# Strided sparse attention and a rational MLP on one core: the whole program re-expressed as a dependency graph with a list schedule

## Chip, cores and metric

One core of a Trainium2 chip. The metric is device time in microseconds of one execution. The engines are TensorE (PE), VectorE (DVE), ScalarE (ACT), GpSimd (POOL) and SyncE (SP, which here only issues DMAs).

## The reference

Attention over `q`, `k`, `v` of shape (8 batches, 8 heads, 576 positions, 64), then an MLP on all 4608 tokens:

```
scores = (1/8) * q @ k.T
heads 0-3: keep 0 <= i-j < 32;  heads 4-7: keep j <= i and i % 32 == j % 32
x = softmax(scores) @ v          # heads concatenated: (4608, 512)
h = x @ w_in                     # (4608, 2048)
g = (a0 + a1 h + a2 h^2 + a3 h^3) / (1 + |b0||h| + |b1| h^2 + 1e-6)
out = g @ w_out                  # (4608, 512) float32
```

## The kernel before

Everything is bfloat16 on chip with float32 in PSUM. POOL casts q and k of a batch into DRAM scratch (L304, one DMA for a pair of heads) and v straight into SBUF (L289); SP then loads q and k transposed, a pair of heads per DMA (L316, L320). Three batches of v and four of q and k are cast ahead.

`attn_head` (one head) goes over five tiles of 128 keys. Scores stand with keys on partitions: a matmul of kT and qT (L371), a matmul that adds the mask through an identity (L384), Exp on ACT without a row maximum (L391), and matmuls with v (L407) that sum over key tiles in one PSUM bank; the 65th column of v is ones, so the row sum comes along. Local heads take some 192 or 256 queries per key tile, strided heads all queries from the key tile on, masked. DVE divides, one reciprocal and one multiplication for each block of tokens (L435, L443), into token tiles X of 128 rows. When a tile has all heads, SP transposes it in four DMAs of 128x128 (L481) into XT, 512 tokens to a chunk.

`mlp1` runs a chunk: 16 groups of four matmuls (L507), each copied out by ACT (L516). Then the Padé chain on 4 pieces of 2048 columns: seven DVE operations for denominator and numerator (L532 to L563), Ln and Exp(-x) on ACT as the division (L573, L581), two DVE operations for the product (L589, L594). `mlp2` runs four blocks of 16 matmuls with w_out into one PSUM bank (L626), copied by DVE (L636), stored by POOL (L645). There is one set of chain buffers (`NCS = 1`).

The order on each engine is the order in which the build loop emits: per batch eight heads, after each head one step of the waiting chain (Ln after head 5, Exp after head 6, the products after head 7), then the transposes, then `mlp2` of the last chunk and `mlp1` of the next. Each engine runs its list in order and waits on semaphores.

Of the kernel before, what the change touches and what calls it, by code (L numbers as in the profile page):

```python
# [6 lines left out]
AF = mybir.ActivationFunctionType  # L7

NEG_BIAS = -240.0
STRIDE = 32  # L10
P128 = 128

DEBUG_STAGE = None
ACT_SET_ID = 6
USE_ACT_PRELOAD = True
LIMIT_B = None
LIMIT_H = None
HEAD_LIST = None
CHAIN_G = None
LN_PER_TILE = False  # L20
XT_ON_ACT = False
# [9 lines left out]
class Ev:  # L31
    __slots__ = ("sig", "n")

    def __init__(self, sig, n):
        self.sig = sig
        self.n = n


class Sig:
    def __init__(self, nc, name, step=1):  # L40
        self.sem = nc.alloc_semaphore(name)
        self.step = step
        self.cnt = 0

    def reserve(self):
        self.cnt += 1
        return Ev(self, self.cnt)

    def cur(self):
        return Ev(self, self.cnt)  # L50


class EngQ:
    def __init__(self, name):
        self.name = name
        self.q = []
        self.maxwait = {}

    def waits(self, evs):
        need = []  # L60
        for ev in evs:
            if ev is None or ev.n <= 0:
                continue
            key = id(ev.sig)
            if self.maxwait.get(key, 0) >= ev.n:
                continue
            self.maxwait[key] = ev.n
            need.append(ev)
        return need


def _blocks(b, S):
    res = []
    u0 = b * S
    u_end = (b + 1) * S
    u = u0
    while u < u_end:
        g = u // P128
        u1 = min((g + 1) * P128, u_end)
        res.append((u - u0, u1 - u, g, u % P128))  # L80
        u = u1
    return res


def bass_strided_sparse_attn__then__act_rational_pade_kernel(nc, q, k, v, moe_w_in, moe_w_out, moe_a, moe_b, out):
    w_in, w_out, pa, pb = moe_w_in, moe_w_out, moe_a, moe_b
    B, H, S, D = q.shape
    assert D == 64
# [3 lines left out]
    assert w_in.shape[0] == Fin and w_out.shape[0] == Fmid  # L92
    NT = B * S
    assert out.shape[0] == NT and out.shape[1] == Fout
    assert S % 64 == 0 and NT % P128 == 0
    HL = H // 2

    NKT = (S + 127) // 128
    KT = [(t * 128, min(128, S - t * 128)) for t in range(NKT)]
    NPAIR = H // 2  # L100
    NK1 = Fin // 128
    NK2 = Fmid // 128
    NF = Fmid // 128
# [12 lines left out]
    A = nc.alloc_sbuf_tensor
    bfty = dt.bfloat16
    f32 = dt.float32
    VST = 68
    NLD = 3  # L120
    vb = [A(f"vb{i}", [128, NKT, H, VST], bfty) for i in range(NLD)]
    qs16 = nc.dram_tensor("qs16", [B, NPAIR, S, 128], bfty)
    ks16 = nc.dram_tensor("ks16", [B, NPAIR, S, 128], bfty)
    NQT = 6
    qT = [A(f"qT{i}", [128, NKT * 128], bfty) for i in range(NQT)]
    kT = [A(f"kT{i}", [128, NKT * 128], bfty) for i in range(NQT)]
    NE = 6
    ET = [A(f"ET{i}", [128, 512], bfty) for i in range(NE)]
    NXR = 8
    XR = [A(f"X{i}", [128, Fin], bfty) for i in range(NXR)]  # L130
    NXTS = 2
    XT = [[A(f"XT{c}_{kk}", [128, CH], bfty) for kk in range(NK1)] for c in range(NXTS)]
    NCS = 1
    HB = [A("hbt", [128, NF, CH], bfty)]
    QM = [A("qmt", [128, NF, CH], bfty)]
    LG = [A("lgt", [128, NF, CH], bfty)]
    T3B = [A("t3t", [128, NF, CH], bfty)]
    NLANE = 1
    ch_z = [A(f"chz{i}", [128, G, CH], bfty) for i in range(NLANE)]
# [650 lines left out]
```

How the kernel before makes its waits and increments, by code:

```python
def bass_strided_sparse_attn__then__act_rational_pade_kernel(nc, q, k, v, moe_w_in, moe_w_out, moe_a, moe_b, out):  # L85
# [116 lines left out]
        def thunk(eng, _need=need, _ev=ev, _maker=maker):  # L202
            for w in _need:
                eng.wait_ge(w.sig.sem, w.n * w.sig.step)
            inst = _maker(eng)
            inst.then_inc(_ev.sig.sem, _ev.sig.step)
# [255 lines left out]
    def do_x_transposes(g):  # L462
        xslot = g % NXR
        c = (g * P128) // CH
        cs = c % NXTS
        col0 = (g * P128) % CH
        if DEBUG_STAGE == 'x':
            ev = emit(QPOOL, S_dbg,
                      lambda s, xslot=xslot, g=g: s.dma_start(
                          out[g * 128:g * 128 + 128, 0:min(Fin, Fout)], XR[xslot][:, 0:min(Fin, Fout)]),
                      waits=[X_last_norm[g]])
            QPOOL.q.append(lambda p, ev=ev: p.wait_ge(ev.sig.sem, ev.n * ev.sig.step))
            X_free[xslot] = ev
            xt_done_ev[g] = ev
            return
# [268 lines left out]
    if DEBUG_STAGE is None:  # L744
        while pending_mlp2:
            run_steps(("dve", "ln", "exp"), 10 ** 6)
            mlp2(pending_mlp2.pop(0))
        run_steps(("dve", "ln", "exp"), 10 ** 6)
        while deferred_out:
            deferred_out.pop(0)[1]()
    for so in S_out:
        if so.cnt > 0:
            QPOOL.q.append(lambda p, so=so: p.wait_ge(so.sem, so.cnt * so.step))
    with nc.Block() as block:
        block.sync(lambda e: [f(e) for f in QSP.q])
```

## Time and profile before

| | |
|---|---|
| median of 3 runs (lowest to highest) | 925.08 us (922.75 to 926.25) |
| profiled execution, first to last instruction | 924.9 us |
| mean granted TensorE clock | 0.724 of 2.4 GHz |
| DMA | 180,868 packets, 42.73 MB |

Busy time is the time in which an engine runs instructions; SPq and POOLq are the queues' own work of issuing DMAs, which the page does not count as busy. A chain row is one link of the work that ended last, followed back from the end. Two matmuls in a row overlap, so a single matmul's mean is longer than its share of a row of them. No time of the profiled execution beyond its span is given.

### The profile page before, as it was taken

The page shows a single profiled execution, that of the slowest core. Times are in us where ns is not written, and L with a number is a line of the kernel's source. Part 1 is how long each engine was busy: PE and PEld are TensorE (multiplying, and loading weights), DVE is VectorE, ACT ScalarE, POOL GpSimd, SP SyncE. Part 2 cuts the span into 40 slices and gives each one's busy share as a digit, 9 for nine tenths or more (in the row PEclk, how much of TensorE's full clock was granted, in tenths as well). Part 3 has the DMA queues.
Part 4 walks back from the last instruction along what each step waited for, and adds up shares of the span by engine and source line. Part 5 has one row for each costly group of instructions (what it writes and reads, how often), then busy time and mean ns, then how long its engine had stood idle before and what let it go on. Part 6 is the DMA issues. An engine that isn't in the chain of part 4 may idle for free.

```text
span 924.9 us, 7533 instructions
## 1 busy us (share of the span) xinstructions
PE 593.8 (64%) x2704; PEld 255.2 (28%) x2704; DVE 460.7 (50%) x1001; ACT 345.3 (37%) x569; POOL 154.4 (17%) x167
## 2 busy tenths in 40 slices
PE   0493496469744985499628974698549854915706
PEld 0241142224321342134213432244213421302202
DVE  0131059522954098416941495319540984393681
ACT  0131155406460437124531555053704371261540
POOL 9986000240006000600020000000000000000000
PEclk9999975589556955596559755795569555967959
DMA  9999901490109010931051010101010000100001
GB/s 120 137 156 192 99 19 20 36 116 25 26 8 128 24 26 13 94 71 26 14 49 59 13 26 16 50 24 25 0 46 23 1 1 18 57 0 23 23 0 45
DMA packets 180868, 42.73 MB, mean 46 GB/s; under 512 B 175712, under 2 KB 178016, under 8 KB 180832
## 3 DMA queue, kind: packets, MB, share of 16 engines
q0 software_dynamic: 118016, 27.80, 30.7%
q1 hardware_dynamic: 62816, 14.47, 9.4%
q8 instruction: 21, 0.34, 0.2%
q14 instruction: 15, 0.12, 0.0%
HBM read 36.98 MB, written 18.87 MB: 60 GB/s over the span
## 4 chain that ended last, share of the span: by engine, by line
PE 53%; DVE 23%; ACT 15%; SPq 3%; DMA 2%; issue 2%; POOL 2%; DVEq 0%; POOLq 0%
PE ps_out L626 16%; PE ps_h L507 14%; PE ps_score L371 8%; PE ps_score L384 8%; PE ps_acc L407 7%; ACT lgt L573 7%; ACT qmt L581 5%; DVE lgt L594 5%; DVE chz L589 3%; DVE X L443 3%; ACT ET L391 3%; DVE outsb L636 2%; SPq L481 2%; DVE qmt L543 1%; DVE chu L554 1%
## 5 line engine op out<-in xcount | busy, mean ns | idle before, releaser
L626 PE MATMUL ps_out<-Wout,lgt 128*128 128x512 bf16 x576 | 148.2, 416 | 152.0 <-DVE lgt L594 130.8
L391 ACT ACTIVATE ET<-ps_score 128x192 bf16<-128x192 f32 (+5 forms) x352 | 126.6, 369 | 225.0 <-PE ps_score L384 195.5
L516 ACT ACTIVATE hbt<-ps_h 128x512 bf16<-128x512 f32 x144 | 86.0, 597 | 309.4 <-PE ps_h L507 309.4
L435 DVE RECIPROCAL rcol<-ps_acc 128x1 f32<-128x1 f32 (+1 forms) x320 | 51.1, 160 | 268.5 <-PE ps_acc L407 266.8
L407 PE MATMUL ps_acc<-vb,ET 128*128 128x65 bf16 (+3 forms) x784 | 127.0, 244 | 79.0 <-ACT ET L391 76.2
L371 PE MATMUL ps_score<-qT,kT 64*128 64x192 bf16 (+5 forms) x352 | 129.2, 367 | 28.7 <-DMA kT<-ks 28.7
L626 PEld LDWEIGHTS ps_out<-Wout,lgt 128*128 128x128 bf16 x576 | 57.8, 106 | 239.9 <-DVE lgt L594 132.7
L407 PEld LDWEIGHTS ps_acc<-vb,ET 128*128 128x128 bf16 (+3 forms) x784 | 75.7, 118 | 136.1 <-ACT ET L391 99.0
L636 DVE COPY outsb<-ps_out 128x512 f32<-128x512 f32 x36 | 24.9, 692 | 151.6 <-PE ps_out L626 151.6
L645 POOL DMA_DIRECT2D out_dram<-outsb x36 | 19.7, 548 | 468.3 <-DVE outsb L636 468.3
L443 DVE TENSOR_SCALAR X<-ps_acc,rcol 128x64 bf16<-128x64 f32 (+1 forms) x320 | 90.8, 284 | 11.4
L289 POOL DMA_DIRECT2D vb<-in_v_dram x40 | 36.3, 939 | 289.2 <-PE ps_acc L407 289.2
L304 POOL DMA_DIRECT2D ks<-in_k_dram x32 | 80.5, 4383 | 4.0 <-issue 4.0
L384 PE MATMUL ps_score<-MS,IDN 128*128 128x512 bf16 (+2 forms) x192 | 78.1, 407 | 0.9
L304 POOL DMA_DIRECT2D qs<-in_q_dram x32 | 77.0, 3952 | 3.4 <-issue 3.4
L573 ACT ACTIVATE lgt<-qmt,consts 128x2048 bf16<-128x2048 bf16 x36 | 69.4, 1990 | 15.9 <-DVE qmt L543 15.9
L507 PE MATMUL ps_h<-XT_0,Win 128*128 128x512 bf16 x144 | 55.3, 384 | 28.9 <-DMA XT_3<-X 28.9
L581 ACT ACTIVATE qmt<-lgt 128x2048 bf16<-128x2048 bf16 x36 | 65.6, 1896 | 0.0
L507 PE MATMUL ps_h<-XT_1,Win 128*128 128x512 bf16 x144 | 55.3, 384 | 0.0
L507 PE MATMUL ps_h<-XT_2,Win 128*128 128x512 bf16 x144 | 55.3, 384 | 0.0
L507 PE MATMUL ps_h<-XT_3,Win 128*128 128x512 bf16 x144 | 55.3, 384 | 0.0
L371 PEld LDWEIGHTS ps_score<-qT,kT 64*128 64x128 bf16 (+1 forms) x352 | 36.5, 104 | 65.6 <-DMA kT<-ks 28.8
(27 smaller groups left out, 496.6 us busy)
## 6 DMA issues: line engine op xcount, KB each, us to landing
out_dram<-outsb POOLq DMA_DIRECT2D x36, 256.0 KB, 2.3
qs<-in_q_dram POOLq DMA_DIRECT2D x32, 144.0 KB, 9.2
ks<-in_k_dram POOLq DMA_DIRECT2D x32, 144.0 KB, 9.5
vb<-in_v_dram POOLq DMA_DIRECT2D x32, 128.0 KB, 4.7
Win<-in_moe_w_in_dram POOLq DMA_DIRECT2D x4, 512.0 KB, 16.5
Wout<-in_moe_w_out_dram POOLq DMA_DIRECT2D x16, 128.0 KB, 22.0
XT_0<-X SPq DMA_TRANSPOSE x36, 3.1
XT_1<-X SPq DMA_TRANSPOSE x36, 2.4
```

Source lines behind the costliest of these rows:

```text
L304: lambda p, b=b, pair=pair, src_t=src_t, dst_t=dst_t: p.dma_start(dst_t[b, pair, :, :].rearrange("s (hh d) -> s hh d", hh=2), src_t[b, 2 * ...
L371: e.matmul(ps[0:nk, 0:x1 - x0], kT[tslot][pbase:pbase + 64, tk0:tk0 + nk], qT[tslot][pbase:pbase + 64, x0:x1], start=True, stop=False),
L384: e.matmul(ps[0:nk, 0:W], IDN[0:nk, 0:nk], mrhs, start=False, stop=True),
L391: a.activation(ET[esl][0:nk, 0:W], ps[0:nk, 0:W], AF.Exp, scale=0.125),
L407: return e.matmul(acc[rb:rb + M, VST * j:VST * j + 65], ET[esl][0:nk, ov0 - x0:ov0 - x0 + M], vb[slot][0:nk, ktile, h, 0:65], start=False, ...
L435: d.reciprocal(rcol[rl][r0:r0 + ns, 0:1], acc[r0:r0 + ns, VST * j + 64:VST * j + 65]),
L443: d.tensor_scalar(XR[xslot][r0:r0 + ns, h * D:(h + 1) * D], acc[r0:r0 + ns, VST * j:VST * j + 64], rcol[rl][r0:r0 + ns, 0:1], None, op0=Al ...
L507: e.matmul(psh[:, 0:CH], Win[kk][:, f * 128:(f + 1) * 128], XT[cs][kk][:, 0:CH], start=(kk == 0), stop=(kk == NK1 - 1)),
L516: a.activation(hbT[:, f, :], psh[:, 0:CH], AF.Copy),
L573: lambda a, qmT=qmT, lgT=lgT, f0=f0: a.activation(lgT[:, f0:f0 + G, :], qmT[:, f0:f0 + G, :], AF.Ln, bias=eps1_ap, scale=1.0),
L581: lambda a, qmT=qmT, lgT=lgT, f0=f0: a.activation(qmT[:, f0:f0 + G, :], lgT[:, f0:f0 + G, :], AF.Exp, scale=-1.0),
L626: e.matmul(pso[:, 0:Fout], LG[0][:, kk, m * 128:(m + 1) * 128], Wout[kk][:, 0:Fout], start=(kk == 0), stop=(kk == NK2 - 1)),
```

## The change

The order is no longer written by hand. Each step is put down as an `Op` with an engine, an assumed duration, a priority key (tokens) and the tiles it reads and writes; `schedule` plays the graph through with these durations, at each engine taking the ready step with the smallest key, and so fixes each engine's list at build time; `emit` writes the lists with the waits that are needed. The lists are static: each engine still runs its own in order.

Attention now has queries on partitions. A local head is six tiles of 96 queries by 128 keys, in two PSUM banks; strided heads go in pairs, each as six blocks by two parities of 54x54 (three residues of 18 tokens). Masks are put in first by matmul; DVE takes the row maximum, TensorE subtracts it through an identity, ACT does one Exp for the unit, SP transposes the probabilities from SBUF, TensorE multiplies with v, and DVE divides with one reciprocal and one multiplication. There are four local units and two strided ones per batch. Strided results go through DRAM (`xs16`, written by POOL) to be reordered; x is transposed by SP from SBUF (local, 256 columns at once) and from DRAM (strided). v is cast into DRAM and loaded by SP, 6 loads for local and 32 for strided heads per batch.

The MLP's chain runs in groups of 8 x 512 = 4096 columns, two per chunk, in rings of 6 (h), 2 (z) and 2 (u) buffers; its formulas are the same. Output blocks are copied by ACT instead of DVE. All casts of all batches depend on nothing and go out as early as their keys let them. Everything of the old body, `Sig`, `EngQ` and `_blocks` is removed. The core of what is added (a step's arguments after its function are assumed duration, key, reads `r`, writes `w`, changes `m`, and assumed transfer time `dma`):

```diff
+            t, e = best
+            while pend[e] and pend[e][0][0] <= t:
+                _, k, i, o = heapq.heappop(pend[e])
+                heapq.heappush(avail[e], (k, i, o))
+            _, _, o = heapq.heappop(avail[e])
+            free[e] = t + o.dur
+            if o.dma is not None:
+                dmafree = max(dmafree, t + o.dur) + o.dma
+                o.fin = dmafree + 2.2
+            else:
+                o.fin = t + o.dur
...
+                lat = 0.07 if u.eng == o.eng else 0.15
+                u.ready = max(u.ready, o.fin + lat)
...
+    R_pL = ring("pL", 3, [128, NTL * 128])
+    R_pS = ring("pS", 2, [128, 2 * NBK * 64])
+    R_ptL = ring("ptL", 2, [128, NTL, TQ])
+    R_ptS = ring("ptS", 2, [128, 2 * 3, 128])
...
+    R_xt = ring("xt", 3, [128, NK1, CH])
+    R_h = ring("h", 6, [128, G, CH])
+    R_z = ring("z", 2, [128, G, CH])
+    R_u = ring("u", 2, [128, G, CH])
...
+    R_ps = Ring([Tile(f"ps{i}", ps(f"ps_s{i}", [128, 2, 512])) for i in range(2)])
+    R_pa = Ring([Tile("pa0", ps("ps_acc", [128, 512]))])
+    R_ph = Ring([Tile(f"ph{i}", ps(f"ps_h{i}", [128, 512])) for i in range(2)])
+    R_po = Ring([Tile("po0", ps("ps_out", [128, 512]))])
...
+    def casts(b):
+        key = b * 576 - 1500 if b else -1e5
...
+        def local(pair):
+            for s_t, d_t in ((q, lq), (k, lk)):
+                P.op("pool", lambda e, s_t=s_t, d_t=d_t: e.dma_start(
+                    d_t[b, pair, :, :].rearrange("s (hh d) -> s hh d", hh=2),
+                    s_t[b, 2 * pair:2 * pair + 2, :, :].rearrange("hh s d -> s hh d")),
+                    4.0, key, w=[T_lqk[b]], dma=2.4)
...
+        def bulk(s_t, d_t, h0, t):
+            n = (H - h0) * S * D
+            c = 1024
+            P.op("pool", lambda e: e.dma_start(
+                bass.AP(tensor=d_t, offset=b * n, ap=[[c, n // c], [1, c]]),
+                bass.AP(tensor=s_t.tensor, offset=s_t.offset + (b * H + h0) * S * D, ap=[[c, n // c], [1, c]])),
+                1.2, key, w=[t], dma=0.9 * (H - h0) / 4)
...
+    def loads(b):
+        key = b * 576 - 700
...
+                P.op("sp", lambda e, t=t, d_t=d_t, pair=pair: e.dma_start_transpose(t.t[:, 0:S], d_t[b, pair, :, :]),
+                     0.15, key + pair, r=[T_lqk[b]], w=[t], dma=0.85)
...
+        for i in range(NTL):
+            w0 = max(0, TQ * i - STRIDE)
+            P.op("sp", lambda e, i=i, w0=w0: e.dma_start(
+                vl.t[:, i, :, 0:64], vs[b, 0:HL, w0:w0 + 128, :].rearrange("h p d -> p h d")),
+                0.15, key + 5, r=[T_v[b]], w=[vl], dma=0.7)
...
+                P.op("sp", lambda e, t=t, d_t=d_t, h=h: e.dma_start_transpose(
+                    t.t[:, h, 0:S // 2], d_t[b, h, :, :].rearrange("(c two) d -> c (two d)", two=2)),
+                    0.15, key + 10, r=[T_sqk[b]], w=[t], dma=0.43)
...
+                P.op("sp", lambda e, i=i, par=par, blk=blk, base=base: e.dma_start(
+                    vS.t[base:base + 52:3, blk // 2, par, :, blk % 2, 0:64],
+                    bass.AP(tensor=vs, offset=((b * H + HL) * S + 2 * i + par) * D,
+                            ap=[[32 * D, TT], [S * D, HL], [1, D]])),
+                    0.15, key + 12, r=[T_v[b]], w=[vS], dma=0.1)
...
+        for kind, idx in (("L", 0), ("S", 0), ("L", 1), ("S", 2), ("L", 2), ("L", 3)):
+            key = base + 96 * u
+            u += 1
+            sc = R_ps.next()
...
+                    for j, n in ((0, 4), (1, 2)):
+                        e.matmul(pst[0:TQ, j, 0:n * 128], IDN[:, 0:TQ], ML[:, j * 512:j * 512 + n * 128],
+                                 start=True, stop=False, skip_group_check=True)
...
+                    for i in range(NTL):
+                        w0 = max(0, TQ * i - STRIDE)
+                        c0 = (i % 4) * 128
+                        r = e.matmul(pst[0:TQ, i // 4, c0:c0 + 128],
+                                     tq.t[pb_:pb_ + 64, TQ * i:TQ * i + TQ], tk.t[pb_:pb_ + 64, w0:w0 + 128],
+                                     start=False, stop=True, skip_group_check=True)
+                    return r
...
+                flat = pst[0:TQ, :, :].rearrange("p a (t c) -> p (a t) c", c=128)[:, 0:NTL, :]
+                P.op("dve", lambda e, flat=flat, ng=ng: e.tensor_reduce(
+                    ng.t[0:TQ, 0:NTL], flat, axis=AX.X, op=Alu.max, negate=True), 0.97, key, r=[sc], w=[ng])
...
+                        r = e.matmul(pst[0:TQ, j, 0:n * 128], IDN[0:TQ, 0:TQ],
+                                     ng.t[0:TQ, 4 * j:4 * j + n].unsqueeze(2).broadcast_to([TQ, n, 128]),
+                                     start=False, stop=True, skip_group_check=True)
...
+                pp = R_pL.next()
+                P.op("act", lambda e, pp=pp, flat=flat: e.activation(
+                    pp.t[0:TQ, :].rearrange("p (t c) -> p t c", c=128), flat, AF.Exp, scale=0.125),
+                    0.83, key, r=[sc], w=[pp])
+                pt = R_ptL.next()
+                P.op("sp", lambda e, pp=pp, pt=pt: e.dma_start_transpose(pt.t[:, :, :], pp.t[0:TQ, :]),
+                     0.15, key, r=[pp], w=[pt], dma=0.83)
...
+                        r = e.matmul(acc.t[0:TQ, 65 * i:65 * i + 65], pt.t[:, i, :], vl.t[:, i, h, 0:65],
+                                     start=True, stop=True, skip_group_check=True)
...
+                P.op("dve", lambda e, rc=rc, a3=a3: e.reciprocal(rc.t[0:TQ, 0:NTL].unsqueeze(2), a3[:, :, 64:65]),
+                     0.22, key, r=[acc], w=[rc])
+                P.op("dve", lambda e, rc=rc, a3=a3, h=h: e.tensor_tensor(
+                    xl.t[0:TQ, :, 64 * h:64 * h + 64], a3[:, :, 0:64],
+                    rc.t[0:TQ, 0:NTL].unsqueeze(2).broadcast_to([TQ, NTL, 64]), op=Alu.mult),
+                    0.56, key, r=[acc, rc], w=[xl])
...
+                for j in range(2):
+                    e.matmul(pst[:, j, 0:NBK * 64], IDN[:, :], MS[:, :], start=True, stop=False,
+                             skip_group_check=True)
+                for j in range(2):
+                    for blk in range(NBK):
+                        for par in range(2):
+                            kc = tk.t[64 * par:64 * par + 64, idx + j, 3 * blk:3 * blk + 288]
+                            r = e.matmul(pst[64 * par:64 * par + SB, j, 64 * blk:64 * blk + SB],
+                                         tq.t[64 * par:64 * par + 64, idx + j, blk, :],
+                                         kc.rearrange("p (t i) -> p t i", i=16)[:, :, 0:3],
+                                         start=False, stop=True, skip_group_check=True)
...
+                    for g in range(3):
+                        for par, c0, mm in ((0, 0, 64), (1, 64, SB)):
+                            r = e.matmul(acc.t[c0:c0 + mm, 130 * g:130 * g + 130],
+                                         pt.t[0:NR, 3 * j + g, c0:c0 + mm], vS.t[0:NR, g, par, h, :, :],
+                                         start=True, stop=True, skip_group_check=True)
...
+                p0 = 64 * par + i3
+                P.op("pool", lambda e, p0=p0, nb=nb, i3=i3, par=par: e.dma_start(
+                    bass.AP(tensor=xs, offset=(b * S + 2 * i3 + par) * 256, ap=[[32 * 256, TT], [6 * 256, nb], [1, 256]]),
+                    xsb.t[p0:p0 + 52:3, 0:nb, :]), 1.0, base + 500, r=[xsb], w=[T_xs[b]], dma=0.4)
...
+                P.op("sp", lambda e, t=t, r0=r0, n=n, col=col, i=i: e.dma_start_transpose(
+                    t.t[:, 0:2, col:col + n], xl.t[r0:r0 + n, i, :]), 0.15, key + i, r=[xl], w=[t], dma=0.3)
...
+            P.op("sp", lambda e, t=t, r0=r0, n=n, col=col: e.dma_start_transpose(
+                t.t[:, 2:4, col:col + n], xs[b, r0:r0 + n, :]), 0.15, key + 10, r=[T_xs[b]], w=[t], dma=1.5 * n / 512)
...
+        base = c * CH + 1150
+        groups = []
+        for g in range(NG):
+            h = R_h.next()
+            for f in range(g * G, g * G + G):
+                ph = R_ph.next()
+                key = base + f * 16
...
+            P.op("act", lambda e, uu=uu: e.activation(uu, uu, AF.Ln, bias=eps1, scale=1.0),
+                 0.833 * W / 1000 + 0.28, key, r=[T_co], m=[u])
...
+        base = c * CH + 1900
+        for m in range(CH // 128):
+            po = R_po.next()
...
+            P.op("act", lambda e, o=o, po=po: e.activation(o.t[:, :], po.t[:, :], AF.Copy), 0.6, base + m * 60,
+                 r=[po], w=[o])
```

## Rows read from the trace of the kernel before

**Rows 1.** The page: span; then busy us, share and instruction count of each engine
```profile
span 924.9 us, 7533 instructions
...
PE 593.8 (64%) x2704; PEld 255.2 (28%) x2704; DVE 460.7 (50%) x1001; ACT 345.3 (37%) x569; POOL 154.4 (17%) x167
```

**Rows 2.** Windows: busy us (count), granted clock, DMA share in two stretches
```profile
core 0: us, PE busy (x) PEld busy (x) DVE busy (x) ACT busy (x) POOL busy (x), PEclk, DMA share, GB/s
128.00:193.00 65.00, 38.65 (x170) 16.98 (x170) 48.99 (x106) 27.48 (x44) 14.19 (x13) 0.50 0.45 43
193.00:227.00 34.00, 31.50 (x155) 12.92 (x152) 4.43 (x14) 12.13 (x24) 4.00 (x6) 1.00 0.40 57
```

**Rows 3.** Chain that ended last, in order of time: start us, us, what
```profile
208.23 13.83 PE ps_h L507 x64
...
251.14 7.57 ACT lgt L573 x4
...
294.16 3.64 PE ps_out L626 x16
```

**Rows 4.** Lines by shape, DVE chain: busy us, mean ns of one; idle before
```profile
L543 DVE TENSOR_TENSOR qmt<-chu,chz 128x2048 bf16<-128x2048 bf16 x36 | 44.1, 1226 | 1.2
...
L589 DVE TENSOR_SCALAR chz<-t3t,coef 128x2048 bf16<-128x2048 bf16 x36 | 29.8, 829 | 3.5 <-DVE lgt L594 0.5
...
L538 DVE TENSOR_SCALAR chu<-chz,coef 128x2048 bf16<-128x2048 bf16 x36 | 29.3, 813 | 1.3
...
L549 DVE TENSOR_SCALAR chz<-hbt,coef 128x2048 bf16<-128x2048 bf16 x36 | 29.2, 812 | 1.3
...
L558 DVE TENSOR_SCALAR chz<-chu,coef 128x2048 bf16<-128x2048 bf16 x36 | 27.1, 753 | 1.3
...
L532 DVE TENSOR_SCALAR chz<-hbt 128x2048 uint16<-128x2048 uint16 x36 | 24.6, 683 | 7.4 <-ACT hbt L516 6.8
```

**Rows 5.** Lines by shape, DVE in attention and output: busy us, mean ns
```profile
L435 DVE RECIPROCAL rcol<-ps_acc 128x1 f32<-128x1 f32 x256 | 40.8, 159 | 132.9 <-PE ps_acc L407 131.9
...
L636 DVE COPY outsb<-ps_out 128x512 f32<-128x512 f32 x36 | 24.9, 692 | 151.6 <-PE ps_out L626 151.6
```

**Rows 6.** Lines by shape, ACT: busy us, mean ns of one; idle before
```profile
L516 ACT ACTIVATE hbt<-ps_h 128x512 bf16<-128x512 f32 x144 | 86.0, 597 | 309.4 <-PE ps_h L507 309.4
...
L573 ACT ACTIVATE lgt<-qmt,consts 128x2048 bf16<-128x2048 bf16 x36 | 69.4, 1990 | 15.9 <-DVE qmt L543 15.9
...
L581 ACT ACTIVATE qmt<-lgt 128x2048 bf16<-128x2048 bf16 x36 | 65.6, 1896 | 0.0
...
L391 ACT ACTIVATE ET<-ps_score 128x512 bf16<-128x512 f32 x32 | 18.8, 588 | 40.3 <-PE ps_score L384 40.3
```

**Rows 7.** Timeline of SP's queue: start us, us, engine, line, operation
```profile
1.16 0.42 SPq L218 DMA_DIRECT2D MS<-c_ms  x1
1.62 0.42 SPq L219 DMA_DIRECT2D IDN<-c_idn  x1
...
28.59 1.20 SPq L316 DMA_TRANSPOSE qT<-qs  x1
29.84 1.27 SPq L320 DMA_TRANSPOSE kT<-ks  x1
...
85.97 1.23 SPq L481 DMA_TRANSPOSE XT_0<-X  x1
87.24 1.23 SPq L481 DMA_TRANSPOSE XT_1<-X  x1
```

**Rows 8.** Line L481: DMA time from issue to landing
```profile
DMA to landing us min/median/max: 2.2/2.6/11.1
```

**Rows 9.** Timeline of the start: first q/k cast, first score matmul
```profile
13.98 1.50 POOL L304 DMA_DIRECT2D qs<-in_q_dram  x1
...
35.87 0.39 PE L371 MATMUL ps_score<-qT,kT 64*128 64x256 bf16 x1 [28.69 <-DMA kT<-ks]
```

**Rows 10.** Chain that ended last, its last wait
```profile
915.34 3.86 issue
```

More of the change, by code:

```diff
@@ L85, in bass_strided_sparse_attn__then__act_rational_pade_kernel, with __init__, next @@
+class Ring:
+    def __init__(self, tiles):
+        self.tiles = tiles
+        self.i = 0
+    def next(self):
+        t = self.tiles[self.i % len(self.tiles)]
+        self.i += 1
+        return t.new()
 def bass_strided_sparse_attn__then__act_rational_pade_kernel(nc, q, k, v, moe_w_in, moe_w_out, moe_a, moe_b, out):
@@ L211, in _act_table_preload, with sb, ring @@
-    def _act_table_preload(a):
+    G = 8
+    NG = NF // G
+    TQ = 96
+    NTL = S // TQ
+    TT = S // STRIDE
+    NBK = 6
+    SB = 3 * TT
+    NR = 64 + SB
+    bf = dt.bfloat16
+    f32 = dt.float32
+    u16 = dt.uint16
+    P = Prog(nc)
+    def sb(name, shape, ty=bf):
+        return nc.alloc_sbuf_tensor(name, shape, ty)
+    def ring(name, n, shape, ty=bf):
+        return Ring([Tile(f"{name}{i}", sb(f"{name}{i}", shape, ty)) for i in range(n)])
+    lq = nc.dram_tensor("lq16", [B, 2, S, 128], bf)
@@ new lines, in bass_strided_sparse_attn__then__act_rational_pade_kernel @@
+    ki = np.arange(128)[None, :]
+    ml = np.full((128, NTL, 128), NEG, np.float32)
+    for i in range(NTL):
+        d = qi - ki if i == 0 else qi + STRIDE - ki
+        ml[:, i, :] = np.where((d >= 0) & (d < STRIDE), 0.0, NEG)
+    ms = np.full((128, NBK, 64), NEG, np.float32)
+    for half in (0, 64):
+        for a in range(SB):
+            for c in range(SB):
+                if a % 3 == c % 3 and c // 3 <= a // 3:
+                    ms[half + a, 0:5, c] = 0.0
+                    if a % 3 == 0:
+                        ms[half + a, 5, c] = 0.0
+            if a % 3:
+                ms[half + a, 5, a] = 0.0
@@ new lines, in mlp2, with mm @@
+    def mlp2(c, groups):
+        base = c * CH + 1900
+        for m in range(CH // 128):
+            po = R_po.next()
+            for g in range(NG):
+                def mm(e, m=m, g=g, po=po):
+                    r = None
+                    for j in range(G):
+                        kk = g * G + j
+                        r = e.matmul(po.t[:, :], groups[g].t[:, j, m * 128:(m + 1) * 128], Wout[:, kk, :],
+                                     start=(kk == 0), stop=(kk == NF - 1))
+                    return r
+                P.op("pe", mm, 0.216 * G, base + m * 60, r=[groups[g], T_wout], w=[po])
+            o = R_o.next()
+            P.op("act", lambda e, o=o, po=po: e.activation(o.t[:, :], po.t[:, :], AF.Copy), 0.6, base + m * 60,
+                 r=[po], w=[o])
+            u0 = c * CH + m * 128
+            dst = Tile(f"st{o.name}") if not hasattr(o, "st") else o.st
+            o.st = dst
+            dst.new()
+            P.op("pool", lambda e, o=o, u0=u0: e.dma_start(out[u0:u0 + 128, :], o.t[:, :]), 0.6, base + m * 60,
+                 r=[o], w=[dst], dma=0.9)
@@ L212, in _act_table_preload, with table @@
+    casts(0)
+    weights()
+    for b in range(1, B):
+        casts(b)
+    nxt = 0
+    st = loads(0)
+    pend = []
+    for b in range(B):
+        cur = st
+        if b + 1 < B:
+            st = loads(b + 1)
+        xl = attention(b, cur)
+        gather(b, xl)
+        while nxt < NCH and (nxt + 1) * CH <= (b + 1) * S:
+            gr = mlp1(nxt)
+            mlp2(nxt, gr)
+            nxt += 1
+    P.schedule()
+    def table(a):
         inst = mybir.InstLoadActFuncSet(name=nc.get_next_instruction_name(), ins=[], outs=[],
-                                         act_func_set_id=ACT_SET_ID)
+                                        act_func_set_id=ACT_SET_ID)
```

1105 lines of the change are left out of this document (430 added, 675 removed).

## The prediction

> **What bounds the kernel now.** I read the page's busy times first, then the windows of one period, then the chain that ended last. The page shows that no engine is full: TensorE is busy 64% of 924.9 us, DVE 50%, ACT 37% [rows 1]. So the span is made of turns. The chain shows whose: in one period the 64 matmuls of a chunk's first layer run alone for 13.83 us, later four Ln take ACT 7.57 us before anything of that chunk can go on, later four blocks of 16 output matmuls run alone at 3.64 us each [rows 3]; the next chunk starts only behind them, because each chunk has one buffer for its whole Padé chain. The windows show the two faces of the period: 65 us with attention and the Padé chain together, in which DVE is busy 49.0 us and TensorE is granted 0.50 of its clock (1.2 GHz), then 34 us of dense matmuls at 1.00 (2.4 GHz) with DVE busy 4.4 us [rows 2]. The gain to be had is to let DVE work in those 34 us; the question is what then becomes the limit. The profiled execution's span is 924.9 us, the median of the runs 925.08 us: the sum below is made against the span and 0.2 us more changes nothing. About 0.5% is what a measurement of this kernel can tell from no change.
>
> **The parts, by engine.** All counts come from the diff; a batch is 576 tokens, a chunk 512, so a batch has 1.125 chunks.
>
> *DVE, Padé chain.* Before, a piece of 2048 columns takes four tensor-tensor operations of 1226 ns and five tensor-scalars of 829, 813, 812, 753 and 683 ns, 8.79 us [rows 4]. The same nine now run on 4096 columns. Fixed cost of one: the 128x1 reciprocal's 159 ns [rows 5]. So one group costs 2 x 8.79 - 9 x 0.159 = 16.2 us (17.6 us if nothing is saved), 18 groups 291 us, with gaps 297 us. Before it was 36 x 8.79 = 317 us.
>
> *DVE, attention.* The row maximum does not exist in the trace. The nearest row is the copy of 128x512 out of PSUM, 692 ns, against 159 ns for one column: 1.04 ns a column [rows 5]. A maximum over 768 columns is then 0.96 us, over 648 columns 0.83 us, a normalisation of 384 columns 0.56 us and a reciprocal 0.17 us. A batch has four local heads (0.96 + 0.17 + 0.56) and two strided pairs (0.83 + 2 x 0.73): 11.3 us, with gaps 11.9 us, 95 us in all. Bounds for the maximum: free of the second bank's latency 0.7 us, twice the copy 1.4 us, which moves the total by +-20 us. The output copies go to ACT. DVE total: 297 + 95 + some 10 us of memsets at the start = 402 us, 49 us a batch.
>
> *ACT.* Ln 1990 ns and Exp 1896 ns at 2048 columns, against 588 ns at 512, give 0.85 ns a column [rows 6]; at 4096 they cost 3.7 and 3.6 us. Per chunk 2 x 7.3 + 16 x 0.597 + 4 x 0.6 = 26.6 us; attention has 4 x 0.80 + 2 x 0.70 = 4.6 us a batch. Sum 276 us, 35 us a batch. It stays off the bound.
>
> *TensorE.* The two layers keep their 1152 matmuls of 512 columns. At full clock they cost 13.83/64 = 0.216 and 3.64/16 = 0.228 us each [rows 3], 256 us together; at half clock 0.427 us, 492 us. Attention has per batch 4 x 2694 + 2 x 4392 = 19,560 columns, 8.2 us at 2.4 GHz and 16.3 us at 1.2 GHz, plus some 4 us for 144 short instructions. So a batch needs 43 us of TensorE at full clock, 81 us at half clock. The mean granted clock decides; the windows show it low whenever attention's short matmuls are in the stretch and high when the 512-column ones run alone [rows 2]. Here both are mixed all the time. I take a mean of 0.75, about 57 us a batch, with TensorE waiting little.
>
> *SP's queue.* This is the part the change's own costs leave out: schedule() prices every SP step at 0.15 us. The trace prices a DMA transpose at 1.20 to 1.27 us and start to start 1.25 to 1.27 us, for 576x128 from DRAM and 128x128 from SBUF alike; a plain DMA takes 0.46 us start to start [rows 7]. The change issues per batch 4 + 8 transposes of q and k, 6 of the probabilities, about 7 + 2 of x (217 in all, 208 before), and now also 6 + 32 plain loads of v that POOL issued before as 5. That is 27 x 1.27 + 38 x 0.46 = 52 us a batch, 416 us in all, where before they cost 264 us with nothing close behind. SP is the fullest queue, and it is in order: a transpose of probabilities that waits for its Exp holds all loads of the next batch, and behind a late transpose wait the value matmul, all of TensorE's matmuls after it, and DVE's normalisation. A unit's way from score to Exp is 1.28 + 0.96 + 0.64 + 0.80 = 3.7 us, plus on average half of a 2.3 us DVE and of a 3.7 us ACT operation that stands in front, 6.7 us; between two such transposes SP has 6 us of other issues. I take 1 us of waiting for each of six units, 58 us a batch. Bounds: none (52), and the whole way uncovered (92).
>
> *Latency.* After issue a transpose lands in 2.6 us (2.2 to 11.1) [rows 8]; schedule() has 2.2 us plus its transfer. This lengthens each unit but two score buffers overlap it; I cost it in the 6.7 us above and not twice. The early casts of all batches keep the DMA engines full for some 150 us, so the upper figure will be met there.
>
> *POOL.* It casts a third as many small pieces, adds 4 gather copies and 6 writes of x a batch, roughly 15 us a batch; nothing waits for it but the xs transposes, whose cover is the next batch's attention. Cost nothing; without the cover about 3 us for each of 8 batches.
>
> *Start.* First cast to first score took 21.9 us, with eight casts to wait for [rows 9]. Now four, issued at 1.4 us instead of 14.0: between 12 and 23 us, I take 18.
>
> *End.* Chunks 7 and 8 both need batch 7, so two chunks of the Padé chain stand behind SP's last transposes: 2.6 us landing, 8 x 4 x 0.216 = 6.9 us of matmuls, 4 x 16.2 = 64.7 us of DVE, then four output blocks with a copy each, 17.0 us, then the last store's issue and 3.9 us of final wait [rows 10]: 96 us.
>
> **Sum:** 18 + 8 x 58 + 96 = 578 us.
>
> **Rivals.** *DVE is the bound (474 us).* If SP's waits are covered and its order runs ahead, DVE does its 402 us with holes only at the start (18 us, and 33 us while batch 0 has nothing for the chain) and the end (21 us). For it: DVE needs 49 us a batch against SP's 52. Against it: SP's price is measured and its order was made with 0.15 us.
>
> *TensorE stays at half clock (695 us).* 492 us of layers and 8 x 20 us of attention, plus 18 and 25 us of ends. For it: 0.50 was granted through 65 us in which TensorE showed 38.7 us busy [rows 2], and the new order puts a wait on ACT or DVE between most groups of matmuls. Against it: in a bound TensorE the long matmuls come back to back, as in the 34 us at 1.00. The Trainium skill, TensorE: Matmul & The Clock Gate, section "A second HAM failure mode: psum-queue depth-cycling", says that short idles between groups that cycle through PSUM banks keep the clock swinging between the levels. That rule speaks against this change, whose first layer has two banks and output one; the rows show only the two pure cases.
>
> *Slower than before (974 us): wide SBUF transposes are paid by blocks.* The probabilities are transposed 96x768 at once, x 96x256; the trace has only 128-column sources. If SP spends 1.27 us for each 128 columns, a batch has 36 + 14 + 4 + 12 = 66 blocks, 84 us, plus 17.5 us of loads and the 6 us of waits, 107.5 us, and 18 + 860 + 96 = 974 us. It turns the sign from 1.27 us a block even without waits (101.4 us a batch). For it: no row excludes it. Against it: 576 rows cost no more than 128 [rows 7]. The Trainium skill, DMA: Bandwidth & Descriptors, section "Why a DMA increments its semaphore by 16 and not by 1", tables a transpose from SBUF on earlier generations at 262,144 cycles for 8,192 tiles, so growing with its tiles; it would point this way, gives no size of a tile and so no time, and no run here shows it yet.
>
> That the change might not do what it says, the same serial turns in a new order, I count in the last two: a static order that reality does not follow shows as waits on SP and TensorE.
>
> **Chances.** SP-paced 0.48, DVE-bound 0.20, half clock 0.24, blocks 0.08. The forecast is the likeliest, 578 us. The range 470 to 720 us holds the first case with both bounds of the start and most of the waits (52 to 68 us a batch give 530 to 658), most of the second and most of the third; outside stay blocks and the far ends. Faster by over 0.5%: 0.91; within: 0.02; slower: 0.07.
>
> **What would show it.** Right: SP's queue issuing some 416 us with few idle stretches, transposes at 1.2 to 1.3 us whatever their width; the chain's largest waits for DMA landings of the probabilities; DVE near 400 us busy, 16.2 us a group; a clock between the levels; a stretch of some 95 us at the end without attention. Wrong: SP idle for long while DVE is above 85% busy (DVE-bound); TensorE above 85% busy at 0.50 through the middle (half clock); transposes of probabilities at 5 us or more on SP (blocks).

## The result and the profile after

The changed kernel takes **778.33 us** (median of 4 runs, 776.72 to 781.19) against 925.37 us on the same chip: a ratio of 0.8416 [0.8393, 0.8439]. The forecast was 578 us with a range up to 720. Sign and mechanism were right, the size was not: the queue named as the bound is the bound, but it needs far longer than the sum gave it.

The page of the changed kernel: span, busy time by engine, three of its rows of 40 slices of 19.5 us, and the chain that ended last, by engine and by line.

```profile
span 779.0 us, 6110 instructions
...
PE 395.9 (51%) x2304; PEld 178.2 (23%) x2304; DVE 362.0 (46%) x353; ACT 267.7 (34%) x265; POOL 141.1 (18%) x184
...
DVE  3000130100309104360298086489088959969960
PEclk9999999999997555795579588799579979999988
DMA  9999969218899042232301342352141321301011
...
SPq 49%; PE 18%; DVE 17%; DMA 6%; ACT 4%; issue 4%; POOL 0%; DVEq 0%; ACTq 0%; POOLq 0%
SPq L455 24%; SPq L440 9%; PE ps_out L683 8%; PE ps_h L641 7%; SPq L615 7%; SPq L433 4%; SPq L428 4%; DVE z L666 3%; DVE z L668 3%; DMA ptL<-pL 3%; DVE h L670 2%; DVE u L660 2%; SPq L509 2%; DVE z L667 1%; ACT u L661 1%
```

Against [rows 1] TensorE's share fell from 64% to 51%, DVE's from 50% to 46%. The chain says what the busy shares can't: half of it is SP's queue issuing DMAs, and half of that is one line, L455, the loads of strided v. Next, what one issue of each of SP's lines costs (views of single lines: count, min/median/max ns of one, first and last start, forms):

```profile
L455 SPq DMA_DIRECT2D vS<-v x256: 737/741/1022, 41.6 to 560.5; - x128
...
L433 SPq DMA_DIRECT2D vL<-v x48: 389/507/4978, 28.9 to 573.7; - x48
...
L509 SPq DMA_TRANSPOSE ptL<-pL x32: 1197/1237/4629, 80.1 to 669.7; - x32
...
L564 SPq DMA_TRANSPOSE ptS<-pS x16: 1211/1286/5364, 86.1 to 644.4; - x16
...
L615 SPq DMA_TRANSPOSE xt<-xL x57: 1159/1241/3992, 185.1 to 685.5; - x57
...
L428 SPq DMA_TRANSPOSE lqT<-lq x16: 1146/1263/11241, 11.2 to 527.9; - x16
```

A transpose costs what [rows 7] said, 1.24 to 1.29 us in the middle, at 96x768 as at 128x128. A strided load costs 0.741 us, not the 0.42 of the small plain loads in [rows 7]. The maxima show the other surprise, single issues of 4 to 11 us; the timeline of the changed kernel's SP queue (start us, us) shows the longest, and one batch's 32 loads in a row, 25.09 us or 0.784 us each:

```profile
12.57 1.34 SPq L428 DMA_TRANSPOSE lkT<-lk  x1
13.96 11.24 SPq L428 DMA_TRANSPOSE lqT<-lq  x1
25.24 3.58 SPq L428 DMA_TRANSPOSE lkT<-lk  x1
...
249.80 25.09 SPq L455 DMA_DIRECT2D vS<-v  x32
```

The windows of the changed kernel, cut where the early casts are over and where SP's last transpose has been issued (686.8 us):

```profile
core 0: us, PE busy (x) PEld busy (x) DVE busy (x) ACT busy (x) POOL busy (x), PEclk, DMA share, GB/s
11.00:250.00 239.00, 69.92 (x456) 32.92 (x456) 43.65 (x60) 30.74 (x36) 65.64 (x81) 0.99 0.89 119
250.00:687.00 437.00, 258.28 (x1557) 118.47 (x1558) 249.97 (x243) 185.96 (x181) 57.40 (x76) 0.77 0.28 58
687.00:779.00 92.00, 67.70 (x292) 26.80 (x290) 61.64 (x36) 50.98 (x48) 8.14 (x12) 0.93 0.09 35
```

For 239 us DVE has 43.65 us of work; the chain of the MLP, which is most of DVE's 362 us, hardly begins. In the middle it is busy 57%. Who then waits for whom (the changed kernel's waits: us in total, times, longest; the last three are SP's own):

```profile
DVE rc L522 <- PE ps_acc L516: 188.9, 20, 24.3
...
PE ps_acc L516 <- DMA ptL<-pL: 163.0, 10, 23.8
...
ACT pL L505 <- DMA ptL<-pL: 121.4, 5, 31.3
```
```profile
SPq L509 <- ACT pL L505: 35.3, 5, 17.9
SPq L564 <- ACT h L645: 28.1, 4, 16.7
SPq L509 <- ACT h L645: 22.7, 5, 10.0
```

Ten waits of up to 23.8 us of the value matmul for a transpose of the probabilities. In eight of the ten its issue stands directly behind a row of 15 to 32 strided loads (32 take 25 us) in the same queue. In the other direction SP itself waits for ACT: its order puts transposes ahead of what is then ready.

**Where the 200 us beyond the forecast are.** SP issues from 11.2 to 686.8 us, 675.6 us. Counted issue by issue in its trace, with gaps of up to 0.2 us between two issues taken as part of issuing, it is issuing for 560 us and idle for 115 us (a merged row of the timeline can hold a wait, so the rows can't simply be added). The forecast had 416 and 48. The issues: 256 strided loads 202 us for 118 forecast, +84; 48 local loads 36 for 22, +14; 217 transposes 323 for 276, +47. The idle time: +67. The first transpose came at 11.2 us where 18 stood, -7; the end took 92 for 96, -4. Together +201.

### The profile page after: what moved, and what is told of

Its sections match the earlier page's. It is cut to its first block, busy times and chain, and to the rows that moved or that the text cites. A ratio compares the mean times of both kernels' runs of the same rounds, so it can differ in the third digit from the quotient of the medians.

```text
span 779.0 us, 6110 instructions
## 1 busy us (share of the span) xinstructions
PE 395.9 (51%) x2304; PEld 178.2 (23%) x2304; DVE 362.0 (46%) x353; ACT 267.7 (34%) x265; POOL 141.1 (18%) x184
## 4 chain that ended last, share of the span: by engine, by line
SPq 49%; PE 18%; DVE 17%; DMA 6%; ACT 4%; issue 4%; POOL 0%; DVEq 0%; ACTq 0%; POOLq 0%
SPq L455 24%; SPq L440 9%; PE ps_out L683 8%; PE ps_h L641 7%; SPq L615 7%; SPq L433 4%; SPq L428 4%; DVE z L666 3%; DVE z L668 3%; DMA ptL<-pL 3%; DVE h L670 2%; DVE u L660 2%; SPq L509 2%; DVE z L667 1%; ACT u L661 1%
## 5 line engine op out<-in xcount | busy, mean ns | idle before, releaser
L683 PE MATMUL ps_out<-Wout,h 128*128 128x512 bf16 x576 | 148.3, 411 | 25.6 <-ACT os L688 13.1
L641 PE MATMUL ps_h<-xt,Win 128*128 128x512 bf16 x576 | 144.2, 403 | 22.2 <-ACT h L645 9.4
L645 ACT ACTIVATE h<-ps_h 128x512 bf16<-128x512 f32 x144 | 85.0, 597 | 107.4 <-PE ps_h L641 107.3
L683 PEld LDWEIGHTS ps_out<-Wout,h 128*128 128x128 bf16 x576 | 57.0, 104 | 103.2 <-issue 17.1
L641 PEld LDWEIGHTS ps_h<-xt,Win 128*128 128x128 bf16 x576 | 52.0, 103 | 98.4 <-ACT h L645 30.4
L661 ACT ACTIVATE u<-u,consts 128x4096 bf16<-128x4096 bf16 x18 | 66.6, 3702 | 2.3 <-DVE u L660 2.2
L663 ACT ACTIVATE u<-u 128x4096 bf16<-128x4096 bf16 x18 | 65.1, 3618 | 0.1
L516 PEld LDWEIGHTS ps_acc<-vL,ptL 128*96 128x96 bf16 x192 | 15.6, 155 | 174.1 <-DMA ptL<-pL 166.9
L688 ACT ACTIVATE os<-ps_out 128x512 f32<-128x512 f32 x36 | 21.5, 596 | 98.6 <-PE ps_out L683 98.5
L481 PE MATMUL ps_s<-ML,IDN 128*96 128x512 bf16 x64 | 21.2, 423 | 57.4 <-DMA lkT<-lk 31.8
L390 POOL DMA_DIRECT2D lk<-in_k_dram x16 | 41.4, 3070 | 0.0
L660 DVE TENSOR_TENSOR u<-u,z 128x4096 bf16<-128x4096 bf16 x18 | 41.1, 2286 | 0.3
L670 DVE TENSOR_TENSOR h<-z,u 128x4096 bf16<-128x4096 bf16 x18 | 41.1, 2282 | 0.1
```

What stands on the lines that cost most here:

```text
L390: P.op("pool", lambda e, s_t=s_t, d_t=d_t: e.dma_start(d_t[b, pair, :, :].rearrange("s (hh d) -> s hh d", hh=2), s_t[b, 2 * pair:2 * pair ...
L641: r = e.matmul(ph.t[:, :], Win[:, kk, f * 128:(f + 1) * 128], xt.t[:, kk, :], start=(kk == 0), stop=(kk == NK1 - 1))
L645: P.op("act", lambda e, f=f, ph=ph, h=h: e.activation(h.t[:, f % G, :], ph.t[:, :], AF.Copy), 0.53, key, r=[ph], w=[h])
L660: dv(lambda e, zz=zz, uu=uu: e.tensor_tensor(uu, uu, zz, op=Alu.mult), tt, r=[z], m=[u])
L661: P.op("act", lambda e, uu=uu: e.activation(uu, uu, AF.Ln, bias=eps1, scale=1.0), 0.833 * W / 1000 + 0.28, key, r=[T_co], m=[u])
L663: P.op("act", lambda e, uu=uu: e.activation(uu, uu, AF.Exp, scale=-1.0), 0.833 * W / 1000 + 0.19, key, m=[u])
```

## The experiments

Three theories, as the expectations name them. T1: the price of an issue on SP, above all of the 32 strided loads. T2: the early casts fill the DMA engines and hold SP. T3: the static order, made with SP steps at 0.15 us, makes SP wait. Unless said otherwise an edit is to the changed kernel.

**e1: the same bytes in 16 loads a batch instead of 32.** The cast writes strided v token-major, so that one load takes both parities.
```
-            for par in range(2):
-                P.op("sp", ... vS.t[base:base + 52:3, blk // 2, par, :, blk % 2, 0:64] ...)
+            P.op("sp", ... vS.t[base:base + 52:3, blk // 2, :, :, blk % 2, 0:64],
+                ap=[[32 * HL * D, TT], [D, 2 * HL], [1, D]] ...)
```


> The strided v loads go in 16 instead of 32 DMAs a batch, each twice as large; for that POOL casts strided v token by token, 18,432 more small packets in all. If SP's issue time sets the pace (T1), SP saves 128 x 0.79 = 101 us and the kernel comes to 680 to 700 us. If the DMA engines, full in the first 250 us, set it (T2), the extra packets (some 39 us of 16 engines) keep it at 770 to 800 us. If it is a bad static order made with wrong prices (T3), it stays within 20 us of 778 us.


Measured 699.92 us, ratio 0.7567 [0.7506, 0.7628]. The loads' line in e1:
```profile
L464 SPq DMA_DIRECT2D vS<-vst x128: 737/741/3266, 41.9 to 477.0; - x128
```
Twice the pieces and bytes per load, the same 741 ns. So 128 issues fewer, 101 us of SP at 0.79, gave 78 us, as T1 expected.

**e8: each load cut in two, the same bytes in 64 a batch.**
```
+                for hh in range(0, HL, 2):
+                    P.op("sp", ... par, hh:hh + 2, blk % 2, 0:64] ... [S * D, 2], [1, D]] ...)
```


> As the changed kernel, but each strided v load is cut in two, 64 a batch, the same bytes and packets. T1: SP issues 256 more at 0.74 to 0.79 us, 190 to 202 us, nearly all of it on the path: 930 to 980 us, slower than the kernel before the change. T2: the same packets, so 780 to 800 us. If the price of an issue falls with its size: 780 to 850 us.


Measured 953.75 us, 1.0295 [1.0246, 1.0344]: slower than the kernel before the change. The loads' line in e8, and its chain:
```profile
L456 SPq DMA_DIRECT2D vS<-v x512: 738/741/1597, 41.4 to 742.2; - x171
```
```profile
SPq 59%; DVE 14%; PE 12%; issue 7%; DMA 5%; ACT 2%; POOL 0%; DVEq 0%; ACTq 0%; POOLq 0%
SPq L456 40%; SPq L440 6%; PE ps_out L684 6%; SPq L616 5%; SPq L428 4%; PE ps_h L642 3%; DVE h L671 2%; SPq L433 2%; DMA ptL<-pL 2%; DVE u L661 2%; DVE z L667 2%; DVE z L669 1%; SPq L510 1%; DVE u L659 1%; DVE z L665 1%
```
Half the bytes, again 741 ns. 256 issues more, 202 us of SP at 0.79, cost 175 us, in T1's range again. What these loads cost SP goes by their count, not by their bytes, and from 16 to 64 loads a batch some four fifths of it reach the end (77% and 87%).

**e4: the loads with 16 of their 18 rows.** Two rows of v per residue are left out.
```
-                    vS.t[base:base + 52:3, blk // 2, par, :, blk % 2, 0:64],
+                    vS.t[base:base + 46:3, blk // 2, par, :, blk % 2, 0:64],
...
-                            ap=[[32 * D, TT], [S * D, HL], [1, D]])),
+                            ap=[[32 * D, 16], [S * D, HL], [1, D]])),
```


> Each strided v load brings 16 of its 18 rows (two rows of v in each residue are left as they were, so their share of the strided heads is missing). It asks why such a load costs SP 0.74 us where one of 128 rows costs 0.51 and one of 128 long rows 0.42. If the row count of 18 is what is dear, it falls to 0.42 to 0.55 us and SP saves 50 to 80 us: 705 to 735 us. If it is the number of dimensions or the step of 3 partitions, it stays at 0.70 us or more: 765 to 785 us.


Measured 746.91 us, 0.8063 [0.7998, 0.8127]. The loads' line in e4:
```profile
L455 SPq DMA_DIRECT2D vS<-v x256: 554/595/1657, 41.6 to 523.7; - x128
```
256 issues at 0.595 for 0.741 us are 37 us less, of which 31 us reach the end. Price and time lie between the two expected cases. The row count is part of the price: two rows fewer take off 0.146 us, where 16/18 of 0.741 would be 0.66. Only 18 and 16 rows were run, so whether it is the number itself, or that 16 goes evenly into the core's 16 DMA engines and 18 does not, isn't separated. In e1, e8 and e4 schedule() also makes the order anew, but SP's idle time, counted as above, stays near the 115 us of the changed kernel (121, 99 and 113), so the order is not what moved these times.

**e2: ACT issues the strided loads.**
```
-                P.op("sp", ... 0.15, key + 12, r=[T_v[b]], w=[vS], dma=0.1)
+                P.op("act", ... 0.79, key + 12, r=[T_v[b]], w=[vS], dma=0.1)
```


> All 32 strided v loads a batch are issued by ACT instead of SP; the same transfers. T1: SP loses 201 us of issuing, ACT's queue gains them (268 us busy plus 201), so the kernel comes to 620 to 670 us, with DVE, TensorE and SP near each other. T2: the transfers are the same, 750 to 780 us. T3: 720 to 790 us.


Measured 762.13 us, 0.8239 [0.8178, 0.83], only 16 us less, though 202 us of issues left SP. T1's number was missed; the time lies in the ranges of T2 and T3. The lines of e2: the load on ACT, SP's largest wait behind ACT, and two of ACT's groups with what ended their idle time:
```profile
L455 ACTq DMA_DIRECT2D vS<-v x256: 770/771/5257, 14.8 to 542.6; - x128
```
```profile
SPq L509 <- ACT h L645: 86.5, 12, 19.9
```
```profile
L645 ACT ACTIVATE h<-ps_h 128x512 bf16<-128x512 f32 x144 | 84.2, 597 | 153.0 <-PE ps_h L641 77.3 <-issue 75.6
...
L505 ACT ACTIVATE pL<-ps_s 96x768 bf16<-96x768 f32 x32 | 25.6, 803 | 164.4 <-issue 112.6 <-PE ps_s L499 32.5 <-DMA ptL<-pL 17.5
```
ACT's exponentials now stand behind 25 us of issues (idle "issue" 112.6 us), and SP waits for ACT. The stall changed its queue; it did not go.

**e3: only the prices in the scheduler.** SP's steps are assumed at 1.27 us (transposes), 0.79 (strided v) and 0.55 us (local v). The instructions are the same, in another order.
```
-                     0.15, key, r=[pp], w=[pt], dma=0.83)
+                     1.27, key, r=[pp], w=[pt], dma=0.83)
...
-                    0.15, key + 12, r=[T_v[b]], w=[vS], dma=0.1)
+                    0.79, key + 12, r=[T_v[b]], w=[vS], dma=0.1)
```


> Same instructions; only the order is made anew, with SP's steps at the measured 1.27 us a transpose, 0.79 and 0.55 us a load in place of 0.15 us. T3: with right prices the order fits, below 710 us. T1: SP has the same 580 us to issue, so little, 740 to 780 us. T2: 760 to 780 us.


Measured 725.58 us, 0.7844 [0.7763, 0.7925], 53 us less, between the ranges of T3 and T1. SP's last transpose is out at 627.1 us, 60 us earlier. Counted as above it issues for 553 us (560) and idles for 63 us (115): nearly all of the gain is SP's idle time. SP's three longest waits for ACT in the changed kernel sum to 86 us; in e3 the same pairs show
```profile
SPq L509 <- ACT pL L505: 30.5, 3, 24.4
...
SPq L564 <- ACT h L645: 7.3, 4, 4.0
...
SPq L509 <- ACT h L645: 6.0, 7, 1.5
```
44 us. T3 is a second cause beside T1.

**e5: e1 and e3 together.** 

> Both that helped: 16 strided v loads a batch and the order made with SP's measured prices. If the two act on the same thing, SP's pace, and each takes its own share (issues and waits), the savings of 78 and 53 us add for the most part: 640 to 670 us. If the right prices only helped because SP was overfull, the sum is little better than the first alone: 685 to 700 us.


Measured 657.57 us, 0.7103 [0.7053, 0.7153]: 121 us less, of 131 if both gains added up fully, in the range expected for two separate shares.

**e6: the casts of batch b+2 wait for the local heads' transposes of q and k of batch b (for the last of them).**
```
+        if b + 2 < B:
+            n1 = len(P.ops)
+            casts(b + 2)
+            for o in P.ops[n1:]:
+                o.deps[P.ops[n1 - 1]] = 1
...
-    for b in range(1, B):
-        casts(b)
+    casts(1)
```


> Casts of batch b+2 wait until the transposes of q and k of batch b have landed, where before the casts of all batches went out at once. T2: the early transfers are spread, SP's issues of 2 to 12 us in the first 90 us fall to 1.3 us, the kernel comes to 680 to 720 us. T1: SP still issues 500 us, so at most what its slow issues of the first 90 us cost over their price, some 40 us: 735 to 780 us.


Measured 781.87 us, 0.8453 [0.8415, 0.849], no gain, where T2 had 680 to 720 us. An issue of 11.90 us at the start was still there, and the weights' casts still stood ahead of it.

**e7: e5 with the weights' casts later** (keys -5e4 and -4e4 to -900 and -890). 

> As the run with both, and the weights' casts are put behind those of batch 1 by their keys. If the slow issues of SP between 14 and 60 us come from DMA engines full of weights, the first loads issue at their price and some 20 to 30 us go from the start: 615 to 645 us. If those issues are slow for another reason, or the time is lost again later, within 8 us of the run with both.


Measured 657.39 us, 0.7106 [0.7073, 0.7139], the same as e5. SP's timeline at the start of e5, then of e7; up to the row of 12 strided loads the order of the steps is the same:
```profile
14.63 11.18 SPq L438 DMA_TRANSPOSE lqT<-lq  x1
...
42.19 3.31 SPq L464 DMA_DIRECT2D vS<-vst  x4
45.60 1.15 SPq L450 DMA_TRANSPOSE sqT<-sq  x1
...
67.31 2.93 SPq L518 DMA_TRANSPOSE ptL<-pL  x2
```
```profile
14.41 1.32 SPq L438 DMA_TRANSPOSE lqT<-lq  x1
...
26.32 8.27 SPq L464 DMA_DIRECT2D vS<-vst  x4
34.69 6.88 SPq L450 DMA_TRANSPOSE sqT<-sq  x1
...
55.67 9.64 SPq L464 DMA_DIRECT2D vS<-vst  x12
...
104.78 1.27 SPq L518 DMA_TRANSPOSE ptL<-pL  x1
```
The long issue is gone, 1.32 for 11.18 us, so the place of the weights' casts ahead of it made that one long. But later steps became long instead, four loads 8.27 for 3.31 us and a transpose 6.88 for 1.15, and the row of 12 loads is out at 65.3 us where e5 has it out at 67.3. Of the gain of 10 us 2 are left there. Then the first probabilities are transposed at 104.8 us, in e5 at 67.3: the new order put loads of the next batch ahead of them. What makes an issue long isn't shown. The windows from 14 to 26 us of e5, then of e7:
```profile
14.00:26.00 12.00, 0.00 (x0) 0.00 (x0) 0.00 (x0) 0.00 (x0) 12.00 (x12) 1.00 1.03 198
```
```profile
14.00:26.00 12.00, 2.55 (x10) 1.13 (x10) 0.95 (x1) 0.91 (x1) 9.88 (x14) 1.00 1.55 163
```
By the DMA share (a sum over packets, which can pass 1) the engines were fuller in e7, where the issue was short; by GB/s they were fuller in e5.

**e9 and e10: e5 with loads due later** (key `b * 576 - 700` to `- 100` and `- 300`). 

> As the run with paired loads and prices; only the key of a batch's loads is changed from 700 to 100 tokens ahead. In that run SP issues the loads of batches 0 to 3 before it transposes x of batch 0 at 196 us, and DVE is busy 29 us of the first 200. If the start is lost to this order, x of batch 0 is transposed near 110 us and 50 to 80 us go: 580 to 610 us. If loads that come later then hold up the next batches, some of it comes back: 610 to 650 us. If SP's total alone counts, within 8 us of 658 us.

 

> The same with 300 tokens ahead, between the two. If the order at the start is what counts, 590 to 630 us; if SP's total alone counts, within 8 us of 658 us.


Measured 668.97 us, 0.7223 [0.7198, 0.7249], and 652.35 us, 0.7063 [0.7021, 0.7106]. The first x is transposed at 179.4 and 164.4 us instead of 196.3, so the MLP starts earlier, but the end gains nothing by it: 11 us more than e5 at -100, worse than every case expected, and 5 us less at -300, where the intervals overlap.

**e11 and e12: e10 with gated casts, with and without late weights.** 

> Paired loads, SP's measured prices, loads 300 tokens ahead, weights late, and the casts of batch b+2 held until q and k of batch b are loaded. In the run without the last two the DMA engines are full for some 200 us, and DVE does little until then. If that start is bound by the DMA engines (T2, only there), x of batch 0 is transposed before 140 us and the kernel comes to 600 to 635 us. If it is SP's issuing and the chain of one batch, within 8 us of 652 us.

 

> As the run before it, but the weights are cast early again, so it differs from the run with loads 300 tokens ahead by the hold on the casts alone. If the hold gives the gain of 25 us, 622 to 636 us. If late weights give it, 645 to 656 us. If both are needed, between.


e11 measured **627.52 us** (624.22 to 632.85), 0.6771 [0.6741, 0.6802], the fastest of all, faster than both kernels. Its time is the one expected of a start bound by the DMA engines, but the sign for that did not come: x of batch 0 is transposed at 152.1 us, not before 140, and in the slower e12 at 145.2 us. e12 measured 655.72 us, 0.7084 [0.7048, 0.712], no better than e10. So gated casts give nothing by themselves (e10 to e12), and beside them late weights give 28 us (e12 to e11). Late weights without gated casts were run only with loads 700 tokens ahead (e7, no gain), so that both are needed isn't shown. Windows of e11, its chain, and the first window in e5:
```profile
11.00:250.00 239.00, 101.94 (x672) 47.86 (x679) 79.49 (x96) 57.72 (x62) 74.44 (x89) 0.93 0.98 120
250.00:536.00 286.00, 212.81 (x1310) 100.55 (x1331) 215.40 (x207) 156.87 (x154) 63.55 (x82) 0.86 0.54 88
...
400.00:500.00 100.00, 86.38 (x561) 41.61 (x570) 87.73 (x87) 62.31 (x66) 20.17 (x24) 0.91 0.39 82
```
```profile
PE 27%; DVE 25%; SPq 24%; ACT 8%; issue 8%; DMA 5%; POOL 0%; DVEq 0%; ACTq 0%; POOLq 0%
```
```profile
11.00:250.00 239.00, 69.55 (x464) 33.13 (x464) 52.38 (x65) 37.42 (x39) 87.45 (x95) 0.97 1.18 124
```
SP's share of the chain is down from 49% to 24%, and from 400 to 500 us TensorE and DVE are both busy over 86%. In that stretch the compute engines are the fullest; e5 is already like that there (87% and 86%). What e11 has over e5 is the first part: up to 250 us DVE is busy 79.5 us instead of 52.4. Emptier DMA engines alone don't explain it, since their share up to 250 us is 0.98 in e12 as in e11. That the order which schedule() then finds does it is not tested.

## Why the prediction was right, and wrong

*Right.* **SP's queue as the pacer** (chance 0.48): 49% of the chain, and the time follows the number of its issues in both directions (e1, e8). **Transposes** at 1.27 us whatever their width: medians of 1.24 to 1.29 us, so the rival of 128-column blocks is out. The table in the Trainium skill, DMA: Bandwidth & Descriptors, section "Why a DMA increments its semaphore by 16 and not by 1", that pointed to it is not borne out at these sizes: six times the columns (96x768 for 128x128) cost 1.24 us of issue for 1.23. **Landing** 2.6 us: the probabilities' transposes land in 2.5 us at least, 2.6 in the median. **DVE**: the nine operations of a group sum to 15.6 us for 16.2 forecast; the row maxima, which no row had shown, took 946 and 820 ns for 960 and 830, and the normalisation 549 for 560:
```profile
L660 DVE TENSOR_TENSOR u<-u,z 128x4096 bf16<-128x4096 bf16 x18 | 41.1, 2286 | 0.3
...
L493 DVE TENSOR_REDUCE ng<-ps_s 96x6 bf16<-96x768 f32 x32 | 30.3, 946 | 60.7 <-PE ps_s L487 60.6
...
L547 DVE TENSOR_REDUCE ng<-ps_s 118x12 bf16<-118x648 f32 x16 | 13.1, 820 | 50.5 <-PE ps_s L540 50.5
...
L524 DVE TENSOR_TENSOR xL<-ps_acc,rc 96x384 bf16<-96x384 f32 x32 | 17.6, 549 | 51.2 <-DMA xt<-xs 48.7 <-DMA xt<-xL 2.2
```
DVE came to 362 us (402 forecast), ACT to 267.7 (276). **The end** took 92 us (96), with 61.6 us of DVE in it (64.7). **POOL** has no share of the chain.

*The step that failed: the plain loads of v at 0.46 us an issue, the term 38 x 0.46.* The 0.46 came from single loads of constants [rows 7]. A load of 18 rows into every third partition takes 0.741 us, 0.79 start to start, and 256 of them were 84 us of the 200. They were given one price with the constants although their shape had no row, and so they should have had bounds, which the range did not give them. e8 shows the weight of this number: with 64 such loads a batch the change loses. The range was narrower than the text's own bounds, too: it took "most of the waits", 52 to 68 us a batch, where the whole way uncovered, 92, gives 18 + 8 x 92 + 96 = 850 us. SP took 84 us a batch (675.6 / 8).

*Second: nothing stood for issues that are held.* The text foresaw the DMA engines full "for some 150 us" and costed it in the landing of the transposes alone. In the changed kernel the issues themselves became longer: the transposes took 47 us over their price, 34 us of it outside the probabilities, and the steps before 60 us took 25 us more than the measured prices of 1.27, 0.55 and 0.79 us add up to. That casts in flight are part of the cause e7 shows for one issue; that full DMA engines are the cause isn't shown. **The start** belongs here: the first score came at 31.8 us for 18 (bounds 12 and 23), behind the one issue of 11.24 us; in e7, where that issue is short, it came at 21.5 us.

*Third: "1 us of waiting for each of six units".* SP idled 115 us, over twice the 48 forecast, and 63 in e3, where the order knows the prices. The text named the cause, an order made with 0.15 us, as an argument against DVE as the bound, and put no price on it; it is 53 us.

A small sum is off as well: TensorE at full clock comes to 32 + 8.2 + 4 = 44 us a batch, not 43; nothing hangs on it.

*The rivals.* DVE as the bound is out (46% busy, 57% in the middle); e11 comes nearest to it, with half the loads, a priced order and later casts. TensorE at half clock is out too: busy 51%, with 0.77 granted through the middle and a mean of 0.861 (0.75 was taken), so the turns between attention and layers did not hold it at 0.50. From 244 us on the granted clock goes back and forth between 0.50 and 1.00 (the slices from the 13th on), and this does not set the end. The Trainium skill, TensorE: Matmul & The Clock Gate, section "A second HAM failure mode: psum-queue depth-cycling", describes such a swing; these runs don't show what it swings by here.

*Open.* What in a load's shape makes 0.741 us beside its rows, what holds an issue for up to 11 us, and why late weights pay beside gated casts. Loads of strided v issued by POOL were not tried.

## What to carry to other kernels

Count the issues of each DMA queue and price each by a row of its own shape; in a scheduler that orders a program at build time those prices matter as much as the engines', since a queue believed free is filled with rows of loads that a late transpose then stands behind. Join loads before moving them: the same bytes in half the DMAs gave 78 us, the same DMAs on another in-order engine 16. Take the price of any operation without a row of its own shape as a range, and look first at the one with the largest count.

## What the runs showed of the hardware that was not expected

- The issue of an 18-row load took 0.741 us with 36, 72 or 144 pieces of 128 bytes in it (e8, the change, e1), 0.595 us with 16 rows (e4). ACT needed 0.771 us for the same load.
- One issue lasted 11.18 us in e5 and 1.32 us for the same step where the weights came later (e7), with a DMA share of 1.03 and 198 GB/s in the first case and of 1.55 and 163 GB/s in the second.
